# Loading one attention block's data ahead of the last weight quarters, and reordering the accumulating value loads, in a fused attention and two-layer MLP kernel

## The chip, the cores and the metric

One core of one Trainium2 chip runs the whole program. The time is device microseconds (us) of that core. The median of three runs is what a version is judged by; the profile is of one further execution.

## The reference, cut to what matters

```python
# B, H, S, D = 4, 8, 576, 64; everything float32
q_d, k_d, v_d = (a.reshape(B, H, S // 4, 4, D).mean(axis=3) for a in (q, k, v))
out_up = np.repeat(sm_attn(q_d, k_d, v_d), 4, axis=2)      # "pooled" attention on means of four
mask = np.abs(pos[:, None] - pos[None, :]) < 4             # "local" attention in a narrow band
out_local = softmax(where(mask, q @ k.T / 8, -1e9)) @ v
x = (out_up + out_local) as 2304 tokens x 512
x = (h - tanh(h)) @ moe_w_out,   h = x @ moe_w_in          # w_in 512 x 2048, w_out 2048 x 512
x = (h * cos(h)) @ moe2_w_out,   h = x @ moe2_w_in
```

## The kernel before, in words

The attention is cut into 36 units. A local unit is one block of up to 116 queries of one batch element (five blocks each, 20 local units); a pooled unit is half of the queries and half of the heads of the pooled attention (16). Units 0 to 8 are batch element 0: local 0 to 3, pooled 4 to 7, local 8 (`FIRST = 8`). Units 9, 10 and 11 are the first three local blocks of batch element 1, units 12 to 15 its pooled ones, and so on.

Units 0 to 8 run in a prologue, before or at the very start of the first MLP. All later units are embedded in the first MLP: TensorE (PE) runs 96 steps of it (6 token tiles of 384, times 16 slices of the hidden width), and each step s has two places, 2s and 2s + 1, into which `attention(place)` puts parts of units. Unit 9 + k has its scores (L398 and L403) at place 5k, its transposes at 5k + 3 and its product with the values (`mixes`, L443) at 5k + 4. So unit 9 is scored at place 0 (step 0) and mixed at place 4 (step 2); unit 10 is scored at place 5, in the second half of step 2, and mixed at place 9; unit 11 is scored at place 10, the start of step 5, and mixed at place 14. A step is `attention(2s)`, `hidden(s + 2)` (12 matmuls, L485), `attention(2s + 1)`, `contract(s)` (12 matmuls, L514). The second MLP follows (L485 and L533).

Each local unit needs `qk` (512 KB, L263) and `vb` (256 KB, L270). Units 0, 1, 2, 3 and 8 have a buffer each; units 9, 10, 11 and all later ones share buffer 0. `load_qk(u)` therefore waits until the unit before it in the buffer has been scored, and `load_v(u)` until that unit has been mixed. Both are issued by SyncE (SP), strictly in its program order.

Weights come in quarters: `load_wi(0, n, w_in)` is four DMAs of 256 KB (L282), `load_wo(0, n, w_out)` is one of 1024 KB (L285). Each is split into a high and a low part by ScalarE (ACT) and GpSimd (POOL), or by POOL alone (`lo_of_in`, L995, `split_wo`, L986 and L988, `split_wi`, L979 and L981). A quarter n of w_in is first used by `hidden(4n)`, a quarter of w_out by `contract(4n)`.

SP's order around the change: the loads of unit 9, the first addend of the pooled data of batch element 1 (`load_first_of_four(1)`, L276 and L278, which waits for unit 7 to be mixed), w_out quarter 1, `vb` of unit 9, w_in quarter 2, w_out quarter 2, w_in quarter 3, w_out quarter 3, and then the loop over u from 9, whose first turn loads unit 10.

POOL sums the pooled queries and keys of batch element 0 from the local blocks: `sums_of_block(u, turn)` waits for the block's `qk` and does four operations (L958, L960). Between those of blocks 0 to 3 and 8 it issues two accumulating DMAs for the values, `vd` (L1006) and `v_other` (L1009), then adds the two buffers (L1014). The pooled scores of unit 4 (L412) need all five blocks summed. For batch element 1 POOL issues three rounds of accumulating DMAs (`add_of_four(1, f)`, f = 1, 2, 3; L969 for `qkd`, 576 KB, and L974 for `vd`, 288 KB).

Of the kernel before, what the change touches and what calls it, by code (L numbers as in the profile page):

```python
# [58 lines left out]
FIRST = 8  # L59
LOCALS = [u for u in range(NU) if UNITS[u][0] == "local"]  # L60
LBUF = {u: 0 for u in LOCALS}
# [13 lines left out]
def later_local(u):  # L75
    return min((w for w in LOCALS if w > u), default=None)
# [33 lines left out]
def after(count):  # L110
    return count + CREDIT


def build(nc, qkx, vx, qkf, v4, w_in, w_out, w2_in, w2_out, const, out):
    with ExitStack() as ctx:
# [141 lines left out]
        def _(sp):  # L257
            def load_qk(u):
                _, b, n, _ = UNITS[u]
                i, w = LBUF[u], earlier_in_buffer(u)  # L260
                if w is not None:
                    sp.wait_ge(scored, after(w + 1))
                sp.dma_start(qk[i][:, :], qkx[b, n]).then_inc(qk_ld[i], 16)  # L263

            def load_v(u):
                _, b, n, _ = UNITS[u]
                i, w = LBUF[u], earlier_in_buffer(u)
                if w is not None:
                    sp.wait_ge(mixed, after(w + 1))
                sp.dma_start(vb[i][:, :], vx[b, n]).then_inc(v_ld[i], 16)  # L270

            def load_first_of_four(b):


                sp.wait_ge(scored, after(LAST_POOLED[b - 1] + 1))
                sp.dma_start(qkd[:, :, :].rearrange("p a s -> p (a s)"), qkf[b, :, 0, :]).then_inc(qk_first, 16)  # L276
                sp.wait_ge(mixed, after(LAST_POOLED[b - 1] + 1))
                sp.dma_start(vd[0:QH, :, :].rearrange("p c n -> p (c n)"), v4[b, 0]).then_inc(v_first, 16)  # L278

            def load_wi(m, n, w):  # L280
                for c in range(KC):
                    sp.dma_start(wi_raw[:, n * KC + c, :], w[c * P:(c + 1) * P, n * 512:(n + 1) * 512]).then_inc(wi_ld[m][n], 16)  # L282

            def load_wo(m, n, w):
                sp.dma_start(wo_raw[n][:, :, :], w[n * 512:(n + 1) * 512, :].rearrange("(c p) n -> p c n", p=P)).then_inc(wo_ld[m][n], 16)  # L285

            def store_y(t):
                sp.wait_ge(ev_act, after(2 * t + 2))
                sp.wait_ge(ev_dve, after(2 * t + 2))
                sp.dma_start(y[t], stage[:, :, :].rearrange("p a n -> p (a n)")).then_inc(y_stored, 16)  # L290
# [32 lines left out]
            load_wo(0, 1, w_out)  # L323
            load_v(9)
            load_wi(0, 2, w_in)
            sp.wait_ge(v_added, after(2))
            load_wo(0, 2, w_out)
            load_wi(0, 3, w_in)

            sp.wait_ge(qk_summed, after(4))  # L330
# [4 lines left out]
            for u in range(FIRST + 1, NU):  # L335
                if 5 * (u - FIRST - 1) >= 2 * FC * (next_store + 1):
                    store_y(next_store)
                    next_store += 1
                more = u in LBUF and later_local(u) is not None
                if more:  # L340
                    load_qk(later_local(u))
                if more:
                    load_v(later_local(u))
                for b in range(1, B - 1):

                    if u == LAST_POOLED[b] + 2:
                        load_first_of_four(b + 1)
# [594 lines left out]
        def _(gp):  # L942
# [6 lines left out]
            def sums_of_block(u, turn):  # L949

                i, n = LBUF[u], UNITS[u][2]
                gp.wait_ge(qk_ld[i], 16)
                for hf in range(2):
                    g0, gn, at_ = GROUPS[2 * n + hf]
                    four = qk[i][:, :].rearrange("p (a h k) -> p a h k", a=2 * PAIRS, h=2)[:, :, hf, at_:at_ + FACTOR * gn]
                    four = four.rearrange("p a (g e o) -> p a g e o", e=2, o=2)
                    two = pair_sums[hf][:, :, 0:gn, :]
                    TT(two, four[:, :, :, :, 0], four[:, :, :, :, 1], ALU.add).then_inc(pair_summed, 1)  # L958
                    gp.wait_ge(pair_summed, after(2 * turn + hf + 1))
                    TT(qkd[:, :, g0:g0 + gn], two[:, :, :, 0], two[:, :, :, 1], ALU.add).then_inc(qk_summed, 1)  # L960
# [39 lines left out]
                TT(wo_lo[n][:, c, :], wo_raw[n][:, c, :], wo_hi[n][:, c, :].bitcast(F32), ALU.subtract).then_inc(wo_split, 1)  # L1000


            sums_of_block(0, 0)
            sums_of_block(1, 1)
            gp.wait_ge(v_first, 16)
            gp.dma_start(vd[0:QH, :, :].rearrange("p c n -> p (c n)"), v4[0, 2], accum_op=ALU.add).then_inc(v_accumulated, 16)  # L1006
            sums_of_block(2, 2)
            gp.wait_ge(v_second, 16)
            gp.dma_start(v_other[0:QH, :], v4[0, 3], accum_op=ALU.add).then_inc(v_accumulated, 16)  # L1009
            sums_of_block(3, 3)  # L1010
            sums_of_block(FIRST, 4)
            gp.wait_ge(v_accumulated, 32)
            for c in range(2):
# [69 lines left out]
```

## Time and profile before

| | |
|---|---|
| median of three runs | 926.61 us (926.35 to 927.87) |
| the profiled execution's own time | 929.99 us |
| its span in the trace | 928.1 us |
| PE busy | 908.3 us, 98% |
| VectorE (DVE), ACT, POOL busy | 522.6, 376.2, 145.6 us |
| moved by DMA | 59.57 MB |

PE is the TensorE matmul row; consecutive matmuls overlap in it, so a busy share near 100% says only that PE never stood still. Idle time in front of an instruction is shown in square brackets with what ended it. Times in rows are microseconds from the span's start.

### The profile page before, as it was taken

How to read it: one execution, taken by the hardware profiler on the slowest of the kernel's cores; microseconds unless marked ns; L12 is line 12 of the kernel's file. 1: busy time of each engine (PE TensorE's matmuls, PEld its weight loads, DVE VectorE, ACT ScalarE, POOL GpSimd, SP SyncE). 2: the span in 40 equal slices, each digit the busy share in tenths (PEclk: the TensorE clock that was granted, in tenths of full speed). 3: DMA queues.
4: the chain of work that ended last, by engine and by line, in shares of the span. 5: the costliest groups of instructions: out<-in, count | busy, mean ns of one | idle time of the engine just before them, and what ended most of it. 6: DMA issues, size and time to landing. Idle time of an engine off the chain costs nothing.

```text
span 928.1 us, 15865 instructions
## 1 busy us (share of the span) xinstructions
PE 908.3 (98%) x6264; PEld 842.5 (91%) x6264; DVE 522.6 (56%) x1073; ACT 376.2 (41%) x1055; POOL 145.6 (16%) x167
## 2 busy tenths in 40 slices
PE   7969999999999999999999999999999999999998
PEld 5759999999999999999999999999999899999997
DVE  3733444354445444433334687677777777777765
ACT  4734343443335433432222353443444443443433
POOL 5494600110000100000059830000000000000000
PEclk9989999999999999999999999999999999999999
DMA  9693001562001820020033421000001000000000
GB/s 292 206 278 94 12 2 69 136 144 81 1 1 58 197 71 1 30 75 35 31 129 102 136 70 35 35 1 35 35 0 35 35 1 1 35 1 1 35 1 34
DMA packets 24637, 59.57 MB, mean 64 GB/s; under 512 B 2292, under 2 KB 5492, under 8 KB 24564
## 3 DMA queue, kind: packets, MB, share of 16 engines
q1 hardware_dynamic: 22212, 50.01, 15.9%
q0 software_dynamic: 2352, 8.55, 5.2%
q8 instruction: 49, 0.80, 0.3%
q14 instruction: 24, 0.20, 0.1%
HBM read 49.12 MB, written 9.44 MB: 63 GB/s over the span
## 4 chain that ended last, share of the span: by engine, by line
PE 94%; DMA 3%; SPq 1%; POOL 0%; DVE 0%; ACT 0%; issue 0%
PE ps L485 43%; PE ps L514 22%; PE ps L533 22%; DMA qk<-qkx_in 2%; PE ps L403 2%; PE ps L412 1%; PE ps L443 1%; DMA v_other<-v_in 1%; PE ps L454 1%; PE ps L421 1%; PE ps L427 1%; SPq L282 1%; PE ps L398 0%; PE ps L386 0%; POOL pair_sums L958 0%
## 5 line engine op out<-in xcount | busy, mean ns | idle before, releaser
L485 PE MATMUL ps<-xh,wi_hi 128*128 128x384 f32 x768 | 261.9, 341 | 0.0
L485 PE MATMUL ps<-xh,wi_lo 128*128 128x384 f32 x768 | 258.0, 336 | 0.0
L485 PE MATMUL ps<-xl,wi_hi 128*128 128x384 f32 x768 | 257.4, 335 | 0.0
L485 PEld LDWEIGHTS ps<-xh,wi_hi 128*128 128x128 f32 x768 | 144.2, 188 | 6.9 <-issue 1.2
L485 PEld LDWEIGHTS ps<-xl,wi_hi 128*128 128x128 f32 x768 | 144.2, 188 | 4.0
L485 PEld LDWEIGHTS ps<-xh,wi_lo 128*128 128x128 f32 x768 | 144.1, 188 | 0.0
L637 ACT ACTIVATE gh<-rem 128x384 fp32r<-128x384 f32 x96 | 50.5, 526 | 213.4 <-PE ps L533 142.1
L826 DVE TENSOR_TENSOR ps<-ps,fn 128x384 f32<-128x384 f32 x96 | 54.2, 565 | 142.0 <-ACT fn L625 141.6
L514 PE MATMUL ps<-gh,wo_hi 128*128 128x384 f32 x384 | 133.0, 346 | 0.0
L514 PE MATMUL ps<-gl,wo_hi 128*128 128x384 f32 x384 | 128.8, 336 | 0.0
L514 PE MATMUL ps<-gh,wo_lo 128*128 128x384 f32 x384 | 128.8, 335 | 0.0
L625 ACT ACTIVATE fn<-ps 128x384 f32<-128x384 f32 x96 | 48.5, 505 | 163.1 <-PE ps L485 163.1
L533 PE MATMUL ps<-wo_hi,gl 128*128 128x512 f32 x288 | 113.9, 396 | 0.0
L533 PE MATMUL ps<-wo_lo,gh 128*128 128x512 f32 x288 | 113.7, 395 | 0.0
L533 PE MATMUL ps<-wo_hi,gh 128*128 128x512 f32 x288 | 111.9, 389 | 0.0
L597 ACT ACTIVATE ps<-ps,stats 128x64 f32<-128x64 f32 (+1 forms) x224 | 64.2, 348 | 80.3 <-DVE stats L747 80.3
L842 DVE TENSOR_SCALAR fn<-ps 128x384 f32<-128x384 f32 x96 | 53.4, 556 | 65.4 <-PE ps L485 65.4
L514 PEld LDWEIGHTS ps<-gh,wo_hi 128*128 128x128 f32 x384 | 72.4, 189 | 2.9 <-issue 1.2
L834 DVE TENSOR_TENSOR gl<-ps,gh 128x384 fp32r<-128x384 f32 x96 | 53.3, 556 | 38.6 <-ACT gh L637 38.5
L514 PEld LDWEIGHTS ps<-gh,wo_lo 128*128 128x128 f32 x384 | 72.5, 189 | 0.0
L514 PEld LDWEIGHTS ps<-gl,wo_hi 128*128 128x128 f32 x384 | 72.4, 188 | 0.0
L637 ACT ACTIVATE gh<-ps 128x384 fp32r<-128x384 f32 x96 | 48.4, 505 | 53.2 <-DVE ps L826 52.4
(86 smaller groups left out, 1114.6 us busy)
## 6 DMA issues: line engine op xcount, KB each, us to landing
qk<-qkx_in SPq DMA_DIRECT2D x20, 512.0 KB, 4.7
wi_raw<-w_in_in SPq DMA_DIRECT2D x32, 256.0 KB, 5.5
wo_raw<-w_out_in SPq DMA_DIRECT2D x8, 1024.0 KB, 6.5
qkd<-qkf_in POOLq DMA_DIRECT2D x9, 576.0 KB, 7.6
vb<-vx_in SPq DMA_DIRECT2D x20, 256.0 KB, 3.6
y_between<-stage SPq DMA_DIRECT2D x6, 768.0 KB, 4.4
x<-y_between SPq DMA_DIRECT2D x6, 768.0 KB, 5.0
out<-stage SPq DMA_DIRECT2D x18, 256.0 KB, 2.1
```

What stands on the lines that cost most here:

```text
L282: sp.dma_start(wi_raw[:, n * KC + c, :], w[c * P:(c + 1) * P, n * 512:(n + 1) * 512]).then_inc(wi_ld[m][n], 16)
L403: mm = MM(ps[rows, bank + slot // 4, slot % 4 * KW:(slot % 4 + 1) * KW], qb[i][rows, cols], kb[i][rows, cols], start=False, stop=(slot % 4 ...
L412: mm = MM(ps[0:QH, bank + h4 % 2, (h4 // 2) * SD:(h4 // 2 + 1) * SD], qd[rows, pair, n * QH:(n + 1) * QH], kd[rows, pair, :], start=True, ...
L485: mm = MM(ps[:, h_bank(s), 0:NT], w, xx[:, kc, :], start=(n == 0), stop=(n == last))
L514: mm = MM(ps[:, j, 0:NT], w[:, c % 4, cols], gg[:, :], start=(first and n == 0), stop=(last and n == 2))
L533: mm = MM(ps[:, out_bank(t, j), :], gg[:, cols], w[:, c % 4, :], start=(first and n == 0), stop=(last and n == 2))
L597: e = nc.scalar.activation(src, src, ACT.Exp, scale=scale, bias=negmax[0:n, u % 2, c:c + 1], accum_out=sums_of(u)[:, c:c + 1])
L625: nc.scalar.activation(fn[s % 2][:, :], ps[:, h_bank(s), 0:NT], ACT.Tanh).then_inc(f_done, 1)
L637: nc.scalar.activation(gh[s % 3][:, :], g, ACT.Copy).then_inc(gh_done, 1)
L826: nc.vector.tensor_tensor(h, h, fn[s % 2][:, :], ALU.subtract).then_inc(g_done, 1)
L834: nc.vector.tensor_tensor(gl[s % 3][:, :], g, gh[s % 3][:, :].bitcast(F32), ALU.subtract).then_inc(gl_done, 1)
L842: nc.vector.tensor_scalar(fn[s % 2][:, :], ps[:, h_bank(s), 0:NT], 1.0 / TWO_PI, MAGIC, ALU.mult, ALU.add).then_inc(u_done, 1)
```

## The change: what it does

In SP's program, unit 10's `qk` is issued directly behind w_in quarter 2, that is ahead of w_out quarter 2 and w_in quarter 3; unit 10's `vb` is issued behind w_out quarter 2, ahead of w_in quarter 3. The waits inside `load_qk` (unit 9 scored) and `load_v` (unit 9 mixed) come along with them. The loop's turn for u = 9 then loads nothing.

In POOL's program, the accumulating DMA for `vd` is issued after the sums of block 2 instead of before them, and the one for `v_other` after the sums of block 3 instead of before them. The order of the sums does not change.

```diff
             load_wo(0, 1, w_out)
             load_v(9)
             load_wi(0, 2, w_in)
+            load_qk(FIRST + 2)
             sp.wait_ge(v_added, after(2))
             load_wo(0, 2, w_out)
+            load_v(FIRST + 2)
             load_wi(0, 3, w_in)
...
-                more = u in LBUF and later_local(u) is not None
+
+                more = u > FIRST + 1 and u in LBUF and later_local(u) is not None
...
-            sums_of_block(0, 0)
-            sums_of_block(1, 1)
+            for u in range(3):
+                sums_of_block(u, u)
             gp.wait_ge(v_first, 16)
             gp.dma_start(vd[0:QH, :, :].rearrange("p c n -> p (c n)"), v4[0, 2], accum_op=ALU.add).then_inc(v_accumulated, 16)
-            sums_of_block(2, 2)
+            sums_of_block(3, 3)
             gp.wait_ge(v_second, 16)
             gp.dma_start(v_other[0:QH, :], v4[0, 3], accum_op=ALU.add).then_inc(v_accumulated, 16)
-            sums_of_block(3, 3)
             sums_of_block(FIRST, 4)
             gp.wait_ge(v_accumulated, 32)
```

## Rows read from the trace of the kernel before

**Rows 1.** The chain that ended last: start us, us, what.

```profile
46.79 21.66 DMA qk<-qkx_in
```

**Rows 2.** PE in order of time, embedded units 9, 10 and 11 (start us, us).

```profile
44.73 1.15 PE L403 MATMUL ps<-qk 64*64 64x64 f32 x32
...
68.58 0.77 PE L398 MATMUL ps<-mask_r,eye_r 128*128 128x256 f32 x2 [9.00 <-DMA qk<-qkx_in]
...
74.31 0.33 PE L485 MATMUL ps<-xh,wi_hi 128*128 128x384 f32 x1
...
81.71 0.44 PE L514 MATMUL ps<-gh,wo_hi 128*128 128x384 f32 x1
...
83.91 0.40 PE L398 MATMUL ps<-mask_r,eye_r 128*128 128x256 f32 x2
...
85.31 0.44 PE L485 MATMUL ps<-xh,wi_hi 128*128 128x384 f32 x1
```

**Rows 3.** Stretches: us, busy by engine, then PE's granted clock, DMA share, GB/s.

```profile
62.00:62.50 0.50, 0.00 (x0) 0.00 (x0) 0.00 (x0) 0.00 (x0) 0.50 (x2) 1.00 1.03 258
63.00:63.50 0.50, 0.00 (x0) 0.00 (x0) 0.00 (x0) 0.00 (x0) 0.50 (x1) 0.50 1.01 239
73.00:73.50 0.50, 0.50 (x4) 0.50 (x3) 0.00 (x0) 0.50 (x7) 0.00 (x0) 0.79 1.11 222
...
18.50:19.00 0.50, 0.00 (x0) 0.00 (x0) 0.00 (x0) 0.50 (x7) 0.50 (x2) 0.60 1.31 426
25.00:25.50 0.50, 0.50 (x18) 0.34 (x18) 0.00 (x0) 0.50 (x3) 0.00 (x0) 0.57 1.02 369
```

**Rows 4.** SP's queue in order of time: when each DMA was issued.

```profile
46.20 0.54 SPq L285 DMA_DIRECT2D wo_raw<-w_out_in  x1
...
57.36 0.33 SPq L270 DMA_DIRECT2D vb<-vx_in  x1
71.30 0.33 SPq L263 DMA_DIRECT2D qk<-qkx_in  x1
```

**Rows 5.** Issue to landing: end of w_in quarter 2, then qk of unit 11.

```profile
L282 SPq DMA_DIRECT2D wi_raw<-w_in_in x2: 486/752/1017, 41.4 to 42.0; - x2
DMA to landing us min/median/max: 6.8/7.3/7.7
...
DMA to landing us min/median/max: 8.5/8.5/8.5
```

**Rows 6.** PE in order of time, scores of pooled unit 4.

```profile
19.79 1.24 PE L412 MATMUL ps<-qkd 64*72 64x144 f32 x8 [2.83 <-POOL qkd L960]
```

**Rows 7.** POOL in order of time: sums, accumulating DMAs, weight splits.

```profile
9.11 0.38 POOL L960 TENSOR_TENSOR qkd<-pair_sums 128x112 f32<-128x112 f32 x1
11.03 1.00 POOL L1006 DMA_DIRECT2D vd<-v_in  x1 [1.54 <-DMA vd<-v_in]
...
14.77 0.85 POOL L1009 DMA_DIRECT2D v_other<-v_in  x1 [0.65 <-DMA v_other<-v_in]
15.35 0.90 POOL L958 TENSOR_TENSOR pair_sums<-qk 128x240 f32<-128x240 f32 x1
...
19.29 0.36 POOL L960 TENSOR_TENSOR qkd<-pair_sums 128x104 f32<-128x104 f32 x1
...
25.69 0.87 POOL L1020 TENSOR_TENSOR wi_lo<-wi_raw,wi_hi 128x128 fp32r<-128x128 f32 x2 [1.42 <-ACT wi_hi L656]
...
93.94 0.63 POOL L979 TENSOR_SCALAR wi_hi<-wi_raw 128x512 fp32r<-128x512 f32 x1
```

**Rows 8.** Issue to landing of qk of unit 3, then of unit 8.

```profile
L263 SPq DMA_DIRECT2D qk<-qkx_in x1: 572/572/572, 3.1 to 3.1; - x1
DMA to landing us min/median/max: 9.8/9.8/9.8
...
L263 SPq DMA_DIRECT2D qk<-qkx_in x1: 432/432/432, 4.5 to 4.5; - x1
DMA to landing us min/median/max: 11.7/11.7/11.7
```

## The prediction, as it went on record

> **What bounds the kernel now.** I read the chain of waits first. PE is busy 98% of the span, so the chain is nearly all matmuls, and what matters is where it leaves PE. Apart from start and end it does so for one long piece: the load of unit 10's `qk`, issued at 46.79 us and landing 21.66 us later, at 68.45 [rows 1]. The timeline of PE shows the price: it stood 9.00 us in front of unit 10's scores, from 59.58 to 68.58 [rows 2]. The second place is in the prologue, where PE stood 2.83 us for POOL's last sum of queries and keys [rows 6]. The timeline of PE's waits after 100 us is empty, so nothing later gives or takes time unless a load becomes late. The reader is to see that a DMA bounds the kernel here although the span as a whole is PE's.
>
> The 9.00 us are not all. The granted clock was still 1.00 in 62.00 to 62.50, 0.50 in 63.00 to 63.50, and came back only about 73.2 (0.79 in 73.00 to 73.50) [rows 3]. From 68.58 to 74.31 PE did unit 10's scores and a `contract`: 5.73 us. The same at full clock, around unit 11, is 2.20 (81.71 to 83.91) plus 1.40 (83.91 to 85.31), 3.60 us [rows 2]. The slow clock cost 2.13 us.
>
> **Unit 10's qk.** Its load waits only for unit 9's scores, done at 45.88 [rows 2]; it was issued at 46.79, right behind w_out quarter 3 at 46.20 [rows 4]. So the wait isn't what made it late; 3072 KB of weights ahead of it in SP's queue were. How fast that queue drains can be read: the last piece of w_in quarter 2 was issued at 42.0 and landed up to 7.7 us later, at 49.7 [rows 5]; from there to 68.45 the queue delivered w_out 2, w_in 3, w_out 3 and this `qk`, 3584 KB in 18.75 us, 191 KB/us, while POOL's accumulating loads ran beside it. In the new order the `qk` goes out at 45.9 directly behind w_in quarter 2, and should land at 49.7 + 512/191 = 52.4. PE wants it at 59.58, 7.2 us later. Were it to land at the same offset behind w_out 2 as well, it would be 57.7, still in time. So the 9.00 and the 2.13 go: 11.13 us.
>
> SP, now waiting for unit 9's scores until 45.88, has behind it w_out 2, `vb` of unit 10, w_in 3, w_out 3. W_out 2 goes out at 46.4 instead of before 46.2, which no one feels. The `vb` load waits for unit 9 to be mixed, 57.36 as before [rows 4], and now w_in 3 and w_out 3 (2048 KB, issued before by 46.20) stand behind that wait, until about 57.7 to 60.5. They land near 65 and 70. POOL came to w_in quarter 3 at 93.94 [rows 7]; 12 us earlier is 82, so it is there 17 us ahead.
>
> **Who is late next.** Unit 11's `qk` waits for unit 10's scores, now done at 59.58 + 1.40 = 61.0, and stands behind w_in 3 and w_out 3, which it did not before. Its scores are due at 59.58 + (83.91 - 68.58) - 2.13 = 72.8 [rows 2]. By the rate of 191 KB/us the queue (`qk` 10 and w_out 2) is done at 57.7, and `vb` 10, w_in 3, w_out 3 and `qk` 11, 2816 KB, take 14.7 us more: 72.4. A queue that ran nearly dry adds up to 2 us. So the wait at unit 11 lies between 0 and 1.6; I take 0.8. Since the clock held for 2.9 us of idleness before [rows 3], a wait that short costs no clock. The far bound is the unit's own row before: 8.5 us from issue to landing with no weights ahead, only the third accumulating round in flight [rows 5]. If the last 512 KB take 8.5 instead of 2.7, they land at 78.2, a wait of 5.4.
>
> The Trainium skill (DMA: Bandwidth & Descriptors, Queues, rings and completion order) says that each DMA engine goes round between the queues that have work and drains one queue's packet before the next. Taken as equal shares in bytes it would give SP's queue half of the 258 GB/s of 62.00 to 62.50 [rows 3], 126 KB/us, and unit 11's `qk` a landing 2816/126 = 22.3 us behind 57.7, at 80.0: a wait of 7.2, the clock's 2.13 with it, and 922.9 in place of 914.4. The 191 KB/us that the queue showed say that its share is larger, so the sum stays with them.
>
> **POOL's order in the prologue.** Block 1's sums ended at 9.49. POOL then waited 1.54 us for `vd`, issued at 11.03, later waited 0.65 us, issued at 14.77, and did blocks 3 and 8 from 15.35 to 19.65, 2.15 us each [rows 7]. New order: block 2 from 9.5 to 11.6; `vd` issued until 12.3 (11.03 to 11.79 before); block 3 when its `qk` lands, 3.1 + 9.8 = 12.9 [rows 8], to 15.0; `v_other` issued until 15.6; block 8 when its `qk` lands, 4.5 + 11.7 = 16.2 [rows 8], to 18.3. So the sums are complete at 18.3 instead of 19.65: 1.4 us. PE was waiting for nothing else then [rows 6], and what follows is a chain of PE, DVE and ACT up to `hidden(0)`, so I pass the 1.4 on in full. Bounds: 0, if the accumulating DMAs' shift delays a `qk`; 2.8, the whole wait, if the landings move forward.
>
> The accumulating loads themselves leave up to 0.6 us later. The second one ends the add of the two value buffers, behind which POOL still stood 1.42 us for ACT at 25.69 [rows 7]: hidden.
>
> PE also ran this stretch at half clock: it fell in 18.50 to 19.00 and came back in 25.00 to 25.50 [rows 3]. Shorter idleness, ending at 18.4, could keep the clock or bring it back sooner. From 19.79 to some 25.3 PE's work ran at half clock, 5.5 us; at full clock it would take no less than half of that, so the saving is 2.7 us at most, 0 at least. I take 0.5, near the lower end: under the new order PE is still idle until 18.4, close to where the clock fell.
>
> **Sum.** 9.00 + 2.13 + 1.4 + 0.5 - 0.8 = 12.2 us. The profiled execution took 929.99, so it would take 917.8. The runs' median is 926.61, 3.4 lower than that execution; carried over, 926.61 - 12.2 = 914.4. The 3.4 us can hardly be matmuls at full clock; they may be a shorter stall for the DMA, and then the unprofiled gain is only 8.8.
>
> **Rivals.**
> 1. Forecast: both stalls shrink, unit 11 waits under 3 us. 914.4, own range 911.8 to 917. Chance 0.62.
> 2. The wait moves to unit 11: its `qk` lands at 76 to 80. For: accumulating loads slow a lone `qk` to 8.5 us [rows 5], and 2048 KB now stand ahead. Against: the rate above. A wait of 5.4 with the clock's 2.13 costs 7.5 in place of 0.8: 921.1; at 3.5 without the clock 917.1; at 7.2 with it 922.9. Chance 0.17.
> 3. The runs stall less than the profiled execution: gain 8.8, 917.8. Chance 0.12.
> 4. The prologue keeps its clock: 914.4 + 0.5 - 2.7 = 912.2, the lower part of the forecast's range, 0.1 of its 0.62. The Trainium skill (TensorE: Matmul & The Clock Gate, What's actually happening) says that the point where the gate acts after idleness shifts from run to run, and no run here shows that.
> 5. The change does not do what it says: `qk` 10 still lands after 59.58 because transfers of one queue don't drain in order, by more than 7.2 us. The landings in this trace kept the order closely. It leaves 924 to 926. Chance 0.05, of which 0.03 within 0.2%.
> 6. Slower: unit 11's wait alone eats everything. It needs 13.0 us of cost, so 10.9 of wait plus 2.13 of clock, a landing at 83.7, 22.7 us after its issue at 61.0. The longest in the trace is 21.66, with 3072 KB freshly ahead [rows 1]; here about 2200 KB are left. Chance 0.04.
>
> A measurement of this kernel can tell 0.2%, about 1.9 us. Faster 0.93, within 0.04, slower 0.03. The range for 8 in 10 runs from 911.8, the clock kept and no wait, to 919.5, which takes in rival 3 and half of rival 2.
>
> **What would show it.** PE's row L398 of unit 10 without the 9.00 us, its `qk` landing near 52; SP's queue with `qk` at 45 to 46, `vb` at 56, then w_in 3 and w_out 3; the granted clock at 1.00 from 60 to 75; the wait in front of L412 at about 1.4 instead of 2.83, starting near 18.4. Unit 11's row L398 tells rivals 1 and 2 apart: under 3 us of DMA wait, or more. The prediction is wrong if that wait is over 3, or if POOL stands for w_in quarter 3 or w_out quarter 3.

## The result and the profile after

The changed kernel takes 921.51 us (median of 11 runs, 917.11 to 924.54) against 926.59 for the kernel before (11 runs, 925.25 to 928.61): a ratio of 0.9943, 95% interval 0.9927 to 0.9958. It is faster by 5.1 us where 12.2 were forecast. The profiled execution took 920.63, span 918.8 us. That is 9.3 less than the span of the profiled execution of before, which at 929.99 was slower than all 11 runs of its kernel.

The chain that ended last, in the changed kernel (start us, us, what), beside [rows 1]:

```profile
56.24 15.42 DMA qk<-qkx_in
```

There is again one long DMA in it, and again a `qk`, but of unit 11. PE in order of time, beside [rows 2] and [rows 6]:

```profile
17.20 0.71 PE L415 MATMUL ps<-qkd 64*72 64x144 f32 x8 [1.33 <-POOL qkd L963]
...
33.95 0.44 PE L488 MATMUL ps<-xh,wi_hi 128*128 128x384 f32 x1
...
54.72 0.40 PE L401 MATMUL ps<-mask_r,eye_r 128*128 128x256 f32 x2
...
71.79 0.76 PE L401 MATMUL ps<-mask_r,eye_r 128*128 128x256 f32 x2 [3.72 <-DMA qk<-qkx_in]
...
87.81 0.71 PE L415 MATMUL ps<-qkd 64*72 64x144 f32 x8
```

Unit 10 (54.72) has no wait any more. Unit 11 (71.79) has one of 3.72 us. Stretches of the same execution (us, busy by engine, granted clock, DMA share, GB/s), beside [rows 3]:

```profile
52.00:54.00 2.00, 2.00 (x40) 1.94 (x41) 0.98 (x2) 0.00 (x0) 1.55 (x2) 1.00 0.40 107
...
70.50:71.00 0.50, 0.00 (x0) 0.00 (x0) 0.00 (x0) 0.00 (x0) 0.50 (x1) 0.90 1.11 261
71.00:71.50 0.50, 0.00 (x0) 0.00 (x0) 0.00 (x0) 0.00 (x0) 0.50 (x2) 0.50 0.96 225
...
77.50:78.00 0.50, 0.50 (x4) 0.50 (x3) 0.28 (x2) 0.16 (x2) 0.42 (x2) 0.78 0.07 25
```

The clock fell about 70.9, 2.8 us into the wait, and came back about 77.7. And between 52 and 54 the 16 DMA engines were at 0.40: the queues had all but run empty. SP's queue and the landings, beside [rows 4] and [rows 5]:

```profile
41.25 0.33 SPq L263 DMA_DIRECT2D qk<-qkx_in  x1
41.62 0.43 SPq L285 DMA_DIRECT2D wo_raw<-w_out_in  x1
52.66 0.33 SPq L270 DMA_DIRECT2D vb<-vx_in  x1
53.03 1.86 SPq L282 DMA_DIRECT2D wi_raw<-w_in_in  x4
54.99 0.91 SPq L285 DMA_DIRECT2D wo_raw<-w_out_in  x1
56.24 1.27 SPq L263 DMA_DIRECT2D qk<-qkx_in  x1
```

```profile
L282 SPq DMA_DIRECT2D wi_raw<-w_in_in x4: 432/432/433, 53.0 to 54.5; - x4
DMA to landing us min/median/max: 4.1/8.9/10.5
...
L263 SPq DMA_DIRECT2D qk<-qkx_in x1: 1273/1273/1273, 56.2 to 56.2; - x1
DMA to landing us min/median/max: 15.4/15.4/15.4
```

The 9.3 us between the two profiled executions add up from three places. The MLP's first matmul starts at 33.95 instead of 38.62: 4.67. Unit 10's wait and slow clock: 11.13, as costed. Unit 11's wait, 3.72, and the slow clock behind it: from its first scores to the pooled scores of unit 12 are 71.79 to 87.81, 16.02 us, where the version `qk10_only` below, which has no wait there, takes 68.79 to 82.07, 13.28: 2.74.

```profile
68.79 0.40 PE L400 MATMUL ps<-mask_r,eye_r 128*128 128x256 f32 x2
...
82.07 0.71 PE L414 MATMUL ps<-qkd 64*72 64x144 f32 x8
```

So -4.67 - 11.13 + 6.46 = -9.34.

### The profile page after: what moved, and what is told of

It is laid out like the page before. It is cut to its first block, busy times and chain, and to the rows that moved or that the text cites. A ratio compares the mean times of both kernels' runs of the same rounds, so it can differ in the third digit from the quotient of the medians.

```text
span 918.8 us, 15865 instructions
## 1 busy us (share of the span) xinstructions
PE 906.6 (99%) x6264; PEld 841.5 (92%) x6264; DVE 523.6 (57%) x1073; ACT 376.1 (41%) x1055; POOL 145.1 (16%) x167
## 4 chain that ended last, share of the span: by engine, by line
PE 95%; DMA 2%; POOL 1%; ACT 1%; DVE 1%; issue 0%; SPq 0%
PE ps L488 44%; PE ps L536 22%; PE ps L517 22%; DMA qk<-qkx_in 2%; PE ps L406 2%; PE ps L446 1%; PE ps L457 1%; PE ps L415 1%; PE ps L424 1%; PE ps L430 1%; POOL pair_sums L961 1%; PE ps L401 0%; POOL qkd L963 0%; ACT ps L600 0%; PE ps L389 0%
```

## The experiments

Each time stands beside that of the kernel before on the same chip; ratios are to it, with 95% intervals.

**The same two kernels again.** The kernel before, unchanged:

> The kernel before, unchanged, profiled a second time. Theory A (the profiled execution of before, 929.99 us, stalled longer for unit 10's qk than most runs): its time is near 926.6 and PE's wait in front of unit 10's scores is some 6 us instead of 9.0. Theory B (the 3.4 us are profiling overhead): again near 930 with a wait of 9.

927.55 us, span 925.7. The time is the one that theory A expects, but the wait at unit 10 is 8.74 us, not 6, so A falls: in this pair the stall is not what differs.

```profile
66.49 0.77 PE L398 MATMUL ps<-mask_r,eye_r 128*128 128x256 f32 x2 [8.74 <-DMA qk<-qkx_in]
```

Theory B (again near 930) falls too. 1.81 of the span's 2.4 us are the prologue: the first MLP matmul starts at 36.81 instead of 38.62. The pooled scores of unit 4 start 0.81 sooner, and the half clock behind them ends near 22.4 instead of 25.4, which is the other 1.0.

The changed kernel, unchanged:

> The changed kernel, unchanged, profiled a second time. Its runs span 917.1 to 924.5 us and those with the highest granted clock are the fastest. Theory A (the spread is the length of unit 11's wait for its qk, plus the clock that it loses): the difference in time to the first profile (920.63, wait 3.7, clock loss 2.7) shows up at that wait and nowhere else. Theory B: the spread comes from the prologue, the wait at unit 11 stays at 3.7.

922.64, span 920.8, 2.0 longer than the first profile. The wait at unit 11 was 3.54, and the first MLP matmul started at 36.09 instead of 33.95. This pair supports theory B. Here too a part is the clock: in this second profile it was at half in the prologue, from about 18.1 to 21.5, in the first it stayed up.

**The two parts alone.** `sp_alone` is the changed kernel with POOL's old order (the edit shown), `pool_alone` the kernel before with POOL's new order:

```diff
-            for u in range(3):
-                sums_of_block(u, u)
+            sums_of_block(0, 0)
+            sums_of_block(1, 1)
             gp.wait_ge(v_first, 16)
...
+            sums_of_block(2, 2)
             gp.wait_ge(v_second, 16)
```

> Only SP's part of the change; POOL's order as before. Theory A (the 9 us and the clock's 2.1 at unit 10 go, unit 11 gives back 6 to 7): unit 10 without a DMA wait, unit 11 with one of 3 to 5 us, time 922 to 924. Theory B (POOL's part, by shifting the prologue, is what brings unit 11's load into collision): no wait at unit 11, time near 916.

922.95 us against 926.75, ratio 0.9953 (0.9928 to 0.9978). Unit 11 waits 3.69 us, unit 10 not at all:

```profile
74.37 0.76 PE L401 MATMUL ps<-mask_r,eye_r 128*128 128x256 f32 x2 [3.69 <-DMA qk<-qkx_in]
```

Theory A holds: SP's part alone makes the new wait. With the slow clock behind it (74.37 to 90.59, 16.22 us, less 13.28) it costs 6.6 us, and the gain of 4.4 us (0.47% of 926.75) is what 11.1 less 6.6 leaves.

> Only POOL's part of the change; SP's order as before. Theory A (the prologue gains through the clock that no longer falls, 4.7 us in the profile of the changed kernel): the first hidden matmul starts near 34 instead of 38.6, unit 10 keeps its wait, time near 922. Theory B (only the 1.4 us of POOL's sums): near 925.

925.37 us, ratio 0.9997 (0.9982 to 1.0011): no difference that can be told. Its profile has the first MLP matmul at 35.98 and unit 10's wait at 8.64. This execution also has a wait of 1.3 us in front of later pooled scores, at 329.84, for an accumulating load. Four of the fourteen profiles have such a wait, of 0.9 to 1.8 us near 320, the others none, whatever the order, so it is a part of the spread between executions:

```profile
PE ps L412 <- DMA qkd<-qkf_in: 1.3, 1, 1.3
```

Theory A's 922 lies below the interval, which allows a gain of 1.7 us at most. The 1.4 us of theory B lie within it, but so does no gain at all: the time can't settle that. The MLP's start in this one profile is 0.8 and 2.6 us sooner than in the two of the kernel before.

**Where unit 11's wait comes from.** Three versions of the changed kernel, each with one thing different, six runs each. The kernel before took 927.88 us beside them. `qk10_only`: unit 10's `vb` stays behind the weights, so that SP doesn't stand until unit 9 is mixed before it issues them.

```diff
             load_wo(0, 2, w_out)
-            load_v(FIRST + 2)
             load_wi(0, 3, w_in)
...
-                more = u > FIRST + 1 and u in LBUF and later_local(u) is not None
-                if more:
+                more = u in LBUF and later_local(u) is not None
+                if more and u > FIRST + 1:
                     load_qk(later_local(u))
```

> The changed kernel, but unit 10's vb stays where it was, behind w_in 3 and w_out 3; so SP does not stand until unit 9 is mixed before it issues these weights. Theory A (unit 11's qk is late because 2048 KB of weights leave only 11 us later, right ahead of it): weights issued by 46, unit 11's qk lands before it is due, no wait there, no clock lost, time 915 to 916.5. Theory B (the queue is late as a whole, whatever the order, because POOL's accumulating loads take their share): a wait of over 2 us at unit 11 remains, time 919 to 922.

916.21 us, ratio 0.9870 (0.9845 to 0.9896). No wait at unit 11 (68.79 above), the clock 1.00 throughout. POOL's second round went out at 54.05, so it was in the way here as well. Unit 11's `qk`, issued at 57.12, took 10.0 us and landed 1.7 us before it was due.

`qk11_first`: unit 11's `qk` also ahead of the weights.

```diff
             load_v(FIRST + 2)
+            load_qk(FIRST + 3)
             load_wi(0, 3, w_in)
...
-                if more:
+                if more and u > FIRST + 2:
                     load_qk(later_local(u))
```

> The changed kernel with unit 11's qk also moved ahead of w_in 3 and w_out 3. Theory A: no weights ahead of it, it lands within 9 us of its issue near 57, no wait at unit 11; w_in 3 and w_out 3 land near 72 and POOL reaches them at 79, so no new wait; time 915 to 916.5. Rival: the weights are now late for POOL or the next qk, a wait of some us appears behind it, time over 919.

916.28 us, ratio 0.9879 (0.9845 to 0.9913); five of the six runs lie between 913.67 and 916.52, one is at 922.81. No wait for the `qk`, and none for the later weights: the last of them landed at 72.9, and POOL reached w_in 3 at 78.76.

```profile
L263 SPq DMA_DIRECT2D qk<-qkx_in x1: 328/328/328, 56.8 to 56.8; - x1
DMA to landing us min/median/max: 6.9/6.9/6.9
```

`rounds_later`: SP's order as in the changed kernel; POOL issues its second and third accumulating round later, at 62.56 and 72.11 instead of 53.19 and 63.09.

```diff
-            add_of_four(1, 2)
             split_wo(0, 1)
-            add_of_four(1, 3)
+            add_of_four(1, 2)
             for c in range(KC):
                 lo_of_in(2, c, 13 + c)
+            add_of_four(1, 3)
```

> The changed kernel with POOL's second and third accumulating round each issued one block of weight splits later (second some 8 us later, near 63; third behind w_in 2's split, near 71). Theory B (the accumulating loads beside it are what slows SP's queue): between 53 and 63 the weights run at over 300 KB/us, unit 11's qk lands in time, wait 0 to 1, time 915 to 917. Theory A in its pure form (only the amount ahead counts): the wait stays at 3 us or more, time 920 to 922.

914.83 us, ratio 0.9864 (0.9837 to 0.9890). SP's queue is as in the changed kernel, but what it holds lands sooner:

```profile
L282 SPq DMA_DIRECT2D wi_raw<-w_in_in x4: 432/432/433, 55.1 to 56.5; - x4
DMA to landing us min/median/max: 3.7/4.3/5.3
...
L263 SPq DMA_DIRECT2D qk<-qkx_in x1: 328/328/328, 58.3 to 58.3; - x1
DMA to landing us min/median/max: 8.8/8.8/8.8
```

From the first w_in 3 issue to the landing of `qk` 11 stand 2560 KB in 12.0 us (55.1 to 67.1), 213 KB/us; in the changed kernel the same 2560 KB take 18.6 us (53.03 to 71.66), 137 KB/us. `qk` 11 was due at 69.97, 2.9 us after it landed. The over 300 KB/us of theory B did not come at once: all DMA together moved 226 GB/s in 56 to 58, 280 and 307 in the next two stretches of 2 us. So theory A in its pure form falls: the amount ahead is the same, and the wait is gone. But theory B in its pure form falls with `qk10_only` and `qk11_first`, where POOL's rounds are in the window and no wait is left. Both are needed for the wait: the weights issued late, right ahead of unit 11's `qk`, and POOL's rounds beside them. Which round counts for how much is not separated, since this version moves the second and the third, and both ran beside those 2560 KB in the changed kernel.

**The same for the kernel before.** `later_sp_before` is the kernel before with only POOL's rounds moved, the diff above.

> The kernel before with only POOL's second and third round later; SP's and the sums' order as before. Theory A (3072 KB of weights ahead of unit 10's qk set its landing): PE still waits over 6 us for it, time 923 to 927. Theory B (the accumulating loads beside them do): second round gone from the window, the wait is 4 us or less, time under 922.

923.18 us against 926.95, ratio 0.9957 (0.9939 to 0.9976).

```profile
63.17 0.77 PE L398 MATMUL ps<-mask_r,eye_r 128*128 128x256 f32 x2 [4.82 <-DMA qk<-qkx_in]
```

Unit 10 waits 4.82 us instead of 8.7 to 9.0: between both theories. The second round makes up some four of the nine microseconds. The rest stands with the 3072 KB ahead and the first round, which stayed where it was (45.79); these two were not taken apart.

**The clock by itself.** 16 dummy matmuls in front of unit 11's scores in the changed kernel:

```diff
+                if now == FIRST + 3:
+                    pe.wait_ge(gathered, after(FIRST + 3))
+                    keep_warm(16, 6)
                 if now is not None:
                     scores(now)
```

> The changed kernel with 16 dummy matmuls of 512 columns (3.4 us at full clock) on PE in front of unit 11's scores. If the clock is lost because PE stands there, its 2.7 us come back and the dummies lie inside the wait: 918 to 919.5, and a narrower spread of runs. If the clock falls for another reason, time stays at 921.5; if the wait in most runs is shorter than 3.4, the dummies themselves cost and it is above 922.

920.77 us, ratio 0.9916 (0.9885 to 0.9946), which overlaps that of the changed kernel: inconclusive as a time. Its profile says more. The dummies ran from 69.15 to 72.98, PE then stood 1.83 us, and its scores began at full clock; the clock fell about 76.3, 1.5 us after they began. From unit 11's scores to unit 12's pooled scores it took 14.96 us (74.81 to 89.77), so the slow clock cost 1.7: less than the 2.7 of the changed kernel's first profile, but as much as in its third, below, which has no dummies. In this execution the `qk` needed 16.8 us, so PE lost 5.7 us in front of the scores, dummies included, and nothing was won.

```profile
74.81 0.47 PE L401 MATMUL ps<-mask_r,eye_r 128*128 128x256 f32 x2 [1.83 <-DMA qk<-qkx_in]
...
75.00:76.00 1.00, 1.00 (x28) 0.86 (x29) 0.00 (x0) 0.00 (x0) 1.00 (x2) 1.00 0.00 0
76.00:76.50 0.50, 0.50 (x15) 0.43 (x10) 0.09 (x1) 0.00 (x0) 0.45 (x1) 0.84 0.12 33
76.50:77.00 0.50, 0.50 (x2) 0.50 (x3) 0.50 (x1) 0.00 (x0) 0.47 (x1) 0.50 0.00 0
```

**The last three.** The changed kernel again, beside the next two and `later_sp_before`:

> The changed kernel once more, as the neighbour of the next three. 921 to 923, a wait of 3 to 5 us for unit 11's qk in its profile, and the clock down behind it.

920.09 us against 926.95 (six runs, 915.33 to 923.03), ratio 0.9910 (0.9884 to 0.9937). The median is 1 us below what was expected, and the wait in its profile, 2.61 us, is shorter than expected; the wait and the slow clock cost 4.3 us here (71.05 to 86.01, less 13.28, is 1.68) after 6.46 in the first profile and 6.2 in the second. With this third profile neither theory of `after_look` is enough: the waits were 3.72, 3.54 and 2.61, the starts of the MLP 33.95, 36.09 and 34.32; both vary.

`later_old_sums` is `rounds_later` with POOL's old order of the sums.

> POOL's rounds later as in rounds_later, but POOL's order of sums and value loads in the prologue as before. With no wait at unit 11 the prologue's part shows undisturbed. If the new order of sums is worth the 1.4 us of POOL's waits (and up to 2 more where the clock stays), this is 1 to 3 us above rounds_later's 914.8; if the gain is swallowed before the MLP begins, it is the same within 1.

916.62 us (four runs, 916.37 to 917.20), ratio 0.9884 (0.9866 to 0.9902), first MLP matmul at 35.36. It is 1.8 us above `rounds_later` in time and 0.2% in ratio, as expected for a real gain, but the intervals overlap. `later_and_qk10` joins `rounds_later` and `qk10_only`, new order of the sums.

> POOL's rounds later and unit 10's vb left behind the weights: both cures together. If each alone already removes the whole wait, 914.5 to 916, no better than either; if a small wait was left in some runs of either, the spread narrows and the median is 1 us lower.

915.15 us (four runs, 914.71 to 915.27), ratio 0.9867 (0.9849 to 0.9885). The two cures together are no better than one, but the runs lie within 0.6 us. Against `later_old_sums`, on the same chip, it is 1.5 us faster; the intervals of the ratios overlap, and the two differ in the weights' order as well. In their profiles the spans differ by 1.7 us (912.8 and 914.5): 0.7 is the start of the MLP (34.70 and 35.36), and 0.9 is the late wait of `later_old_sums` for an accumulating load, near 317.

## Why the prediction was wrong

**What bounds the kernel, and unit 10.** Right. The 9.00 us of wait and the 2.13 of slow clock went as costed. Unit 10's `qk` was to land 6.5 us after its issue; it took 5.8 in the profile (41.25 to 47.05) and left 7.7 us of slack where 7.2 were forecast.

**The step that failed: "the wait at unit 11 lies between 0 and 1.6; I take 0.8", and "a wait that short costs no clock".** The mechanism was named and its place was right, but the term measured 3.72 + 2.74 = 6.46 us in the profile, and 6.6 in the SP part alone. That is rival 2, to which I gave 0.17: its band of 917 to 923 holds the measured 921.5, and its landing of 76 to 80 holds the measured one (71.66, which is 76.3 on the time scale of the kernel before, whose MLP starts 4.67 later). Two things made the term small. And it had no room: 72.4 forecast against 72.8 due leaves 0.4 us, so each microsecond by which the queue was slower went into the wait.

First, the rate. I took 191 KB/us from a stretch in which SP's queue was never empty, and treated it as a property of the queue. Unit 9's mixing held SP until 52.66, the queue ran nearly dry (DMA share 0.40 in 52 to 54), and the weights then started together with POOL's second round, issued at 53.19. The last piece of w_in 3 needed 10.5 us from its issue instead of the 5.3 of `rounds_later`. In the terms of the prediction, `qk` 10 and w_out 2 were done at 53.9 (41.62 + 12.3), and the 2816 KB behind them took until 71.66: 17.7 us, 159 KB/us, where the sum had 14.7 us and up to 2 more for a dry queue, for which it had no row.

What the average hid can be read from the bytes that each queue moved. `q1` is what SP issues, `q0` what POOL issues; the profile lists no DMA issued by another engine. The changed kernel in 57 to 63, 63 to 67 and 67 to 72 us:

```profile
q0 software_dynamic: 233, 0.87, 74.2%
q1 hardware_dynamic: 285, 0.53, 27.1%
...
q1 hardware_dynamic: 703, 1.53, 103.7%
q0 software_dynamic: 7, 0.02, 2.2%
...
q0 software_dynamic: 203, 0.79, 78.8%
q1 hardware_dynamic: 178, 0.43, 23.6%
```

(Packets, MB, share of the 16 engines.) While a round's data moved, SP's queue got 0.09 MB/us; between two rounds it got 0.38. The kernel before shows the same two levels, in 51 to 57, 57 to 61 and 61 to 67:

```profile
q0 software_dynamic: 218, 0.85, 72.5%
q1 hardware_dynamic: 332, 0.61, 32.4%
...
q1 hardware_dynamic: 703, 1.41, 99.3%
q0 software_dynamic: 22, 0.04, 4.8%
...
q0 software_dynamic: 218, 0.85, 70.5%
q1 hardware_dynamic: 274, 0.70, 32.2%
```

So 191 KB/us was the mean of about 0.11 MB/us beside a round and 0.35 without one. It holds only for a load that meets the same share of both, and the sum should have asked when the rounds run. The Trainium skill says that a DMA engine alternates between its queues (DMA: Bandwidth & Descriptors, Queues, rings and completion order). Counted in packets the trace roughly agrees: 285 of SP's queue beside 233 of POOL's in 57 to 63, 274 beside 218 in the kernel before in 61 to 67. But SP's packets are half as large there (0.53 MB in 285, against 0.87 in 233). So equal shares in bytes, which is how I had used that rule, is not what the trace shows. Nor is "its share is larger", for which I had set the rule aside: the rate was higher because POOL's rounds pause. The 922.9 that equal shares gave lie only 1.4 above the measured time, but by a wait of 7.2 us where 3.72 was measured, so that closeness is partly luck.

Second, the clock. I read from [rows 3] that 2.9 us of idleness had left the clock up, and took from that that a shorter wait is free. It isn't: see the last section. For the wait that came, 3.72 us, the clock's price was 2.74 where the kernel before had paid 2.13 behind 9.00.

**SP's weights behind the wait.** Right that POOL would not miss them: w_in 3 landed at 65.0 (54.5 + 10.5), w_out 3 at 67.7, and POOL reached w_in 3 at 79.02. On the scale of the kernel before that is 69.7 and 72.4 where 65 and 70 were forecast, so these landings already showed the queue slower than assumed. What was wrong was to look only for who waits for the weights, and to price what they do to the load behind them at the queue's old rate.

**The prologue.** 1.4 + 0.5 were forecast. The nine profiles with the new order of sums have their first MLP matmul at 33.95 to 36.09, mean 35.06; the five with the old order at 35.36 to 38.62, mean 36.95: 1.9 us. The other edits of these versions act only after this stretch, so the fourteen can be compared. The two parts can be told apart by the start of unit 4's pooled scores. It moved from 19.14 to 17.95 on average, 1.2 us where 1.4 were forecast. From there to the first MLP matmul it took 17.81 and now 17.11, 0.7 where 0.5 was forecast, and that part is the clock. In the eight profiles that kept it up this stretch took 16.73 to 17.25 us, in the six in which it fell 17.74 to 18.83. It fell in four of the five with the old order and in two of the nine with the new one. So rival 4, the clock kept, came true in most profiles, though not at its 2.7 us: a fall cost about 1 us, and only the profile that I had read paid 2. These are means of few and scattered profiles. In time the part alone shows 0.9997, at most 1.7 us, and can't be told from nothing.

**Rival 3**, that most runs stall less for unit 10 than the profiled one: two further profiles have 8.74 and 8.64 us, and the versions without any wait gain 1.2 to 1.4%, 11 to 13 us, which speaks against it as well. Where the profiled 929.99 came from is partly seen: 1.8 of it lay in the prologue. **Rivals 5 and 6** did not occur.

The sum with the measured terms: 926.6 - 11.1 - 1.9 + 6.5 = 920.1, 1.4 below the median; that remainder is left open. With the wait removed by any of the three cures the kernel takes 914.8 to 916.3, beside a kernel before at 927.9. By the ratios that is 914.0 to 915.4 on the forecast's scale, which had put it at 914.4.

## What to carry to other kernels

When a load is moved ahead of others in an in-order queue, price the next load behind those others as carefully as the one that was moved: if the moved load carries a wait for compute, everything behind it starts late and in a bunch. A drain rate holds for the backlog and the neighbours it was read with; before using it, split it by what ran beside the queue, ask whether the queue will still be full, and which other queue starts at the same moment. Here a single `qk` ahead, with its `vb` left behind the weights, was worth 1.3% (ratio 0.9870), where both ahead were worth 0.6 to 0.9% (0.9943 and 0.9910).

## What the runs showed of the hardware

A queue's rate has levels, not a mean: SP's queue moved about 0.09 to 0.12 MB/us while an accumulating round of POOL moved its data, and 0.35 to 0.38 MB/us between two rounds, by the six stretches above. A round's data began to move some 2 to 4 us after its issue: of the round issued at 53.19 POOL's queue had moved 0.02 MB by 57.

PE's clock can fall after the wait is over. In `after_timed` PE stood 2.61 us, resumed at 71.05 at full clock, and fell to half about 72.7, with PE fully busy:

```profile
71.05 0.47 PE L401 MATMUL ps<-mask_r,eye_r 128*128 128x256 f32 x2 [2.61 <-DMA qk<-qkx_in]
...
72.00:73.00 1.00, 1.00 (x24) 0.93 (x19) 0.35 (x1) 0.00 (x0) 0.92 (x2) 0.87 0.98 223
73.00:74.00 1.00, 1.00 (x5) 1.00 (x4) 0.51 (x2) 0.42 (x3) 1.00 (x2) 0.50 0.91 131
```

In `fill_at_11` 1.83 us of wait were followed by the same, 1.5 us after its end. Each time it cost 1.7 us. Nor is a longer wait always the dearer one. In the prologue of `after_look` the clock was already down at the end of a wait of 1.40 us, in that of `later_old_sums` it stayed up through one of 1.92 (the stretch from 18.00 of each, and PE's row behind the wait):

```profile
18.35 1.24 PE L415 MATMUL ps<-qkd 64*72 64x144 f32 x8 [1.40 <-POOL qkd L963]
18.00:18.50 0.50, 0.15 (x2) 0.18 (x4) 0.23 (x1) 0.50 (x7) 0.20 (x1) 0.61 1.08 369
...
18.62 0.71 PE L415 MATMUL ps<-qkd 64*72 64x144 f32 x8 [1.92 <-POOL qkd L963]
18.00:18.50 0.50, 0.00 (x0) 0.00 (x0) 0.00 (x0) 0.50 (x7) 0.39 (x2) 1.00 1.06 270
```

So the length of a single wait does not say whether it costs clock. What else decides was not tried.
